# Sliding-window attention with 32-query groups: own 128-key spans and shared global keys instead of 256 score columns a tile

## The reference

```python
# q, k, v: [2, 8, 768, 64]; n_global = 8, n_local = 96
scores = q @ k.T / 8
rel = pos[:, None] - pos[None, :]
is_global = pos[None, :] < n_global
is_local = (rel >= 0) & (rel < n_local)
dist = where(is_global & ~is_local, n_local, abs(rel))
scores = where(is_global | is_local, scores - slope[head] * dist, -1e9)
a = softmax(scores); x = a @ v                  # then [2, 768, 512]
u = x + mix over the sequence (rank 32: U, V)
y = u + relu(u @ w_ch1) @ w_ch2
k2 = relu(shift_k(y) @ w_k); out = sigmoid(shift_r(y) @ w_r) * (k2 * k2 @ w_v)
```

## Time and profile before

| | us |
|---|---|
| Median of three runs | 542.37 (542.26 to 542.88) |
| The profiled execution, its device time | 543.66 |
| Its span in the profile | 541.9 |
| PE busy | 525.9 (97%) |
| DVE, ACT, POOL busy | 196.2, 133.5, 264.8 |
| First score matmul; end of the attention's last weigh | 9.16; 102.19 |

### The profile page before, as it was taken

One profiled execution on the slowest core, in us unless ns is written; L12 is line 12 of the kernel. 1 busy time (PEld: TensorE's weight loads), 2 busy tenths in 40 slices (PEclk: granted clock), 3 DMA queues, 4 the chain that ended last, 5 costly groups with the idle time before them and its releaser, 6 DMA issues.

```text
span 541.9 us, 9496 instructions
## 1 busy us (share of the span) xinstructions
PE 525.9 (97%) x3600; PEld 490.0 (90%) x3600; DVE 196.2 (36%) x529; ACT 133.5 (25%) x288; POOL 264.8 (49%) x282
## 2 busy tenths in 40 slices
PE   3989999999999999999999999999999999999997
PEld 2777787899999999999999999999998998998996
DVE  4866777422322212222122321232342342343223
ACT  2756676311111111111111101112321321321321
POOL 4489454338002700039910369930797797698000
PEclk9999999999999999999999999999999999999999
DMA  8643336002200300004420000000001001001001
GB/s 208 231 151 100 91 88 187 3 0 84 73 0 0 130 26 0 0 0 156 155 77 0 0 1 1 0 0 0 1 1 58 0 0 58 1 0 58 0 0 58
DMA packets 24602, 27.06 MB, mean 50 GB/s; under 512 B 14208, under 2 KB 14208, under 8 KB 24576
## 3 DMA queue, kind: packets, MB, share of 16 engines
q1 hardware_dynamic: 24288, 25.93, 15.0%
q10 hardware_dynamic: 288, 0.79, 0.5%
HBM read 23.57 MB, written 3.15 MB: 49 GB/s over the span
## 4 chain that ended last, share of the span: by engine, by line
PE 92%; POOL 4%; issue 1%; DMA 1%; DVE 0%; POOLq 0%; DVEq 0%
PE bank L500 25%; PE bank L512 25%; PE bank L556 12%; PE bank L565 12%; PE bank L580 6%; PE bank L365 4%; PE bank L398 3%; PE bank L373 3%; PE bank L406 1%; POOL w1l L1012 1%; POOL w2l L1012 1%; DMA v_in<-in_v 1%; PE bank L415 1%; PE bank L412 1%; POOL q_in L967 0%
## 5 line engine op out<-in xcount | busy, mean ns | idle before, releaser
L883 DVE SCALAR_TENSOR_TENSOR HL<-bank,HH 128x384 fp32r<-128x384 f32 x64 | 35.7, 558 | 175.0 <-ACT HH L687 175.0
L687 ACT ACTIVATE HH<-bank 128x384 fp32r<-128x384 f32 x64 | 31.5, 493 | 234.4 <-PE bank L500 234.4
L500 PE MATMUL bank<-UL,w1h 128*128 (+1 forms) x256 | 85.9, 336 | 0.8 <-issue 0.8
L500 PE MATMUL bank<-UH,w1h 128*128 (+1 forms) x256 | 86.4, 337 | 0.0
L512 PE MATMUL bank<-HH,w2h 128*128 128x384 f32 x256 | 86.2, 337 | 0.0
L512 PE MATMUL bank<-HL,w2h 128*128 128x384 f32 x256 | 86.2, 337 | 0.0
L500 PE MATMUL bank<-UH,w1l 128*128 (+1 forms) x256 | 86.1, 336 | 0.0
L512 PE MATMUL bank<-HH,w2l 128*128 128x384 f32 x256 | 85.9, 335 | 0.0
L1010 POOL TENSOR_SCALAR w1h<-raw 128x2048 fp32r<-128x2048 f32 x5 | 9.6, 1922 | 126.2 <-PE bank L512 126.2
L610 ACT ACTIVATE probs<-probs,neg_max 128x256 f32<-128x256 f32 (+1 forms) x96 | 41.0, 480 | 32.8 <-DVE neg_max L768 32.8
L500 PEld LDWEIGHTS bank<-UH,w1h 128*128 128x128 f32 x256 | 48.1, 188 | 1.1 <-issue 1.0
(11 more groups left out here) (110 smaller groups left out, 987.9 us busy)
## 6 DMA issues: line engine op xcount, KB each, us to landing
raw<-in_moe_w_ch SPq DMA_DIRECT2D x8, 1024.0 KB, 6.2
v_in<-in_v SPq DMA_DIRECT2D x8, 384.0 KB, 4.0
out<-result SPq DMA_DIRECT2D x12, 256.0 KB, 2.1
q_in<-in_q SPq DMA_DIRECT2D x7, 384.0 KB, 4.7
k_in<-in_k SPq DMA_DIRECT2D x7, 384.0 KB, 5.4
raw<-in_moe_w_v SPq DMA_DIRECT2D x2, 1024.0 KB, 5.3
raw<-in_moe_w_k SPq DMA_DIRECT2D x2, 1024.0 KB, 5.0
raw<-in_moe_w_r SPq DMA_DIRECT2D x1, 1024.0 KB, 5.6
```

Source lines behind the costliest of these rows:

```text
L500: mm = pe.matmul(bank[4 + f % 2][:, 0:BLK], w[:, kt, f * P:(f + 1) * P], x[:, kt, ds(blk * BLK, BLK)], start=kt == 0 and n == 0, stop=kt = ...
L687: act.activation(HH[:, f % 2, :], bank[4 + f % 2][:, 0:BLK], ACT.Relu).then_inc(hid_high, 1)
L883: dve.scalar_tensor_tensor(out=HL[:, f % 2, :], in0=bank[4 + f % 2][:, 0:BLK], scalar=0.0, in1=HH[:, f % 2, :].bitcast(F32), op0=ALU.max, ...
```

## The change

Each group of 32 queries gets a span of 128 keys of its own (its 32 and the 96 before), read straight from k, which now lies in memory with 96 zero columns ahead; the 32 global keys are scored apart. So a tile has 160 score columns: 32 of globals and 128 of the span. A score matmul has 32 queries as weights and 64 rows: 8 array tiles (2 heads by 4 groups). v comes from memory in four copies, each shifted by 32 rows (`v_in[:, slot, j, t, h, :]`), and the globals' v as `v_glob`; POOL copies neither k nor v any more. The probabilities of the four (tile, head) blocks' global columns are gathered by ACT into one 128x128 block, so that a unit has 5 transpositions. Row sums come from the exponential's accumulator. Scores, transposed blocks and products have two PSUM banks each, without alternation; `scores(n)` waits for the maxima of n-1, and `turn(n)` for both evacuations of n-1.

```diff
-                        mm = pe.matmul(bank[UNIT_BANKS[n % 3][h]][:, at:at + w].rearrange("p (a n) -> p a n", n=P),
-                                       q_in[r, p % 2, t * P:(t + 1) * P], window(p % 2, r, t), start=True, stop=True)
+                if n >= 1:
+                    pe.wait_ge(max_done, 2 * n)
+                for i, t in unit_tiles(n):
+                    for at, w in ((BAND, GLOB), (None, P)):
+                        for j in range(GROUPS):
+                            for h in range(2):
+                                r = slice(h * D, (h + 1) * D)
+                                frm = t * P + j * GROUP if at is None else at
+                                to = i * WIN + (GLOB if at is None else 0)
+                                mm = pe.matmul(bank[SCORE_BANKS[h]][group(j), to:to + w],
+                                               q_in[r, p % 2, t * P + j * GROUP:t * P + (j + 1) * GROUP],
+                                               k_in[r, p % 2, frm:frm + w], start=True, stop=True)
...
+            def turn(n):
+                if n >= 1:
                     for i in range(2):
+                        pe.wait_ge(ptevac[i], n)
                 for h in range(2):
                     pe.wait_ge(exp_done, 2 * n + h + 1)
+                    for i in range(2):
+                        mm = pe.transpose(bank[TURN_BANKS[h]][:, i * P:(i + 1) * P],
+                                          probs[:, n % 2, i, h, GLOB:WIN], ident[:, :])
+                mm.then_inc(pt_done, 1)
+                pe.wait_ge(glob_kept, n + 1)
+                pe.transpose(bank[TURN_BANKS[0]][:, 2 * P:3 * P],
+                             probs_glob[:, n % 2, :], ident[:, :]).then_inc(pt_done, 1)
...
+            def weigh_globals(n):
...
+                for j in range(GROUPS):
+                    for i in range(2):
+                        r = slice(i * 2 * GLOB, (i + 1) * 2 * GLOB)
+                        pe.matmul(WEIGHTED[group(j), i, :], probs_t[r, n % 2, 2, group(j)],
+                                  v_glob[r, p % 2, :, :].rearrange("p h d -> p (h d)"), start=True, stop=False)
+            def weigh(n):
...
+                    for i, t in unit_tiles(n):
+                        for j in range(GROUPS):
+                            mm = pe.matmul(WEIGHTED[group(j), i, h * D:(h + 1) * D],
+                                           probs_t[:, n % 2, turned_at(i, h), group(j)],
+                                           v_in[:, p % 2, j, t, h, :], start=False, stop=h == 1)
...
             def sums_of_x(x):
                 for t in range(ST):
-                    side = slice(t % 2 * 2 * RANK, (t % 2 + 1) * 2 * RANK)
-                    mm = pe.matmul(bank[M_BANK][side, 0:P], U2[:, t, :, :].rearrange("p a r -> p (a r)"), x(t),
+                    for side in (t % 2, t % 2 + 2):
+                        mm = pe.matmul(bank[M_BANK][side * RANK:(side + 1) * RANK, 0:P], U[:, t, :], x(t),
...
             def banded_attention():
-                for n in range(NU + 3):
+                for n in range(1, NU + 3):
                     if 2 <= n < NU + 2:
                         turn(n - 2)
+                    if piece(n) and piece(n)[1] > 0:
+                        mixing(*piece(n))
                     if n < NU:
                         scores(n)
-                    if piece(n):
-                        mixing(*piece(n))
                     if n >= 3:
+                        weigh_globals(n - 3)
+                        if piece(n) and piece(n)[1] == 0:
+                            mixing(*piece(n))
                         weigh(n - 3)
+            scores(0)
```

`scores(0)` now stands ahead of the branch. ACT:

```diff
-                for i, (_, at, w) in enumerate(unit_tiles(n % UNITS)):
-                    pr = probs[:, n % 3, h, at:at + w]
-                    e = act.activation(pr, pr, ACT.Exp, bias=neg_max[:, n % 3, h, i:i + 1], scale=-1.0)
+                for i in range(2):
+                    pr = probs[:, n % 2, i, h, :]
+                    e = act.activation(pr, pr, ACT.Exp, bias=neg_max[:, n % 2, i, h:h + 1], scale=-1.0,
+                                       accum_out=sums[:, n % 4, i, h:h + 1])
                 e.then_inc(exp_done, 1)
+            def keep_globals(n):
+                act.wait_ge(exp_done, 2 * n + 2)
+                act.activation(probs_glob[:, n % 2, :].rearrange("p (a g) -> p a g", g=GLOB),
+                               probs[:, n % 2, :, :, 0:GLOB].rearrange("p i h g -> p (i h) g"),
+                               ACT.Copy).then_inc(glob_kept, 1)
```

```diff
             def load_v(p):
-                sp.dma_start(v_in[:, p % 2, :, :, 0:D], vp[p]).then_inc(v_landed[p % 2], 16)
+                sp.dma_start(v_in[:, p % 2, :, :, :, :], vp[p]).then_inc(v_landed[p % 2], 16)
+                sp.dma_start(v_glob[:, p % 2, :, :], vg[p]).then_inc(v_landed[p % 2], 16)
...
             for p in range(2, PAIRS):
                 sp.wait_ge(qk_done, UNITS * (p - 1))
                 sp.wait_ge(qk_in[p % 2], 32 * (p // 2))
                 load_qk(p)
                 sp.wait_ge(pv_done, UNITS * (p - 1))
-                sp.wait_ge(v_landed[p % 2], 16 * (p // 2))
+                sp.wait_ge(v_landed[p % 2], 32 * (p // 2))
                 load_v(p)
+                if p < 4:
+                    load_chunk(p - 2)
...
+            act.dma_start(q_in[:, 0, 0:FIRST], qt[0][:, 0:FIRST]).then_inc(first_in, 16)
+            act.dma_start(k_in[:, 0, 0:BAND + FIRST], kt_[0][:, 0:BAND + FIRST]).then_inc(first_in, 16)
...
                 for p in range(PAIRS):
                     if p + 2 < PAIRS:
-                        prepare_qk(p + 2)
+                        prepare_pair(p + 2)
                     if p >= 1:
                         split_u(p - 1, 0)
                         split_u(p - 1, 1)
-                    if p + 2 < PAIRS:
-                        prepare_v(p + 2)
-                    if p < 2:
-                        split_chunk(p)
+                    if 1 <= p < 3:
+                        split_chunk(p - 1)
```

More of the change, by code:

```diff
@@ L19, with block_kernel @@
 GLOB = 32
-BAND = P - GLOB
+GROUP = 32
+BAND = P - GROUP
 MASK = 1.0e9
-def block_kernel(nc, qt, kt_, vp, counts, mix_u, mix_v, w_ch1, w_ch2, mus, w_k, w_v, w_r, out):
+def block_kernel(nc, qt, kt_, vp, vg, counts, mix_u, mix_v, w_ch1, w_ch2, mus, w_k, w_v, w_r, out):
     PAIRS, _, S = qt.shape
-    D = vp.shape[4]
+    D = vp.shape[5]
     B, H = out.shape[0], out.shape[2] // D
@@ L143, in block_kernel @@
         v_rows = region("v_rows", [P, S])
-        u_raw = region("u_raw", [P, ST, RANK])
-        region = Region(h_at)
-        dist = region("dist", [P, BCOLS])
-        grid = region("grid", [P, 2 * P])
-        far = region("far", [P, 2 * P])
+        region = Region(y_at)
+        reach = region("reach", [P, 2, WIN])
+        far = region("far", [P, 2, WIN])
+        grid = region("grid", [P, P])
+        place = region("place", [P, P])
+        behind = region("behind", [P, P])
         key = region("key", [P, GLOB])
         glob_far = region("glob_far", [P, GLOB])
+        region = Region(h_at)
+        dist = region("dist", [P, 2, WIN])
+        v_glob = region("v_glob", [P, 2, 2, D])
+        probs_glob = region("probs_glob", [P, 2, P])
         assert region.at <= b_at
@@ L177, in block_kernel @@
         assert end <= nc.sbuf_usable_end, (end, nc.sbuf_usable_end)
[L179 to L183 removed]
+        psum = ctx.enter_context(nc.psum_tensor("psum", [P, 8, 512], F32))
+        bank = [psum[:, i, :] for i in range(8)]
+        WEIGHTED = psum[:, 0:2, 0:2 * D]
+        TURN_BANKS, SCORE_BANKS = (2, 3), (4, 5)
+        M_BANK = 7
         GATE_BANKS = [4, 5, 3]
@@ L333, in _ @@
             sp.dma_start(mu[:, :, :], mus).then_inc(mu_in, 16)
-            for c in range(2):
-                sp.dma_start(raw[c][:, :].rearrange("p (t n) -> p t n", t=4), chunks[c][0]).then_inc(raw_in[c], 16)
             for p in range(2, PAIRS):
@@ L727, in _ @@
                                 -SCALE / slopes[2 * j + h]).then_inc(scale_set, 1)
+            for j in range(GROUPS):
+                dve.memset(group_base[group(j), :], float(j * GROUP)).then_inc(reach_step, 1)
+            reaches()
             dve.wait_ge(counts_in, 16)
@@ L1105 @@
         "q": inputs["q"].transpose(0, 1, 3, 2).reshape(pairs, 2 * d, s),
-        "k": inputs["k"].transpose(0, 1, 3, 2).reshape(pairs, 2 * d, s),
-        "v": inputs["v"].reshape(pairs, 2, tiles, P, d).transpose(0, 3, 2, 1, 4),
+        "k": np.pad(inputs["k"].transpose(0, 1, 3, 2).reshape(pairs, 2 * d, s), ((0, 0), (0, 0), (BAND, 0))),
+        "v": np.zeros((pairs, P, P // GROUP, tiles, 2, d), inputs["v"].dtype),
+        "v_glob": np.zeros((pairs, 2, 2, GLOB, 2, d), inputs["v"].dtype),
         "counts": np.concatenate([np.asarray(inputs[n]).reshape(1) for n in ("n_local", "n_global")]),
     }
+    v = inputs["v"].reshape(pairs, 2, s, d)
+    ahead = np.pad(v, ((0, 0), (0, 0), (BAND, 0), (0, 0)))
+    for j in range(P // GROUP):
```

(5 more changed lines are left out.)

283 lines of the change are left out of this document (124 added, 159 removed).

## The result

The changed kernel takes 568.95 us (567.62 to 570.11, 4 runs) against 542.62 for the kernel before in the same session: ratio 1.0485, 95% interval 1.046 to 1.0509. The forecast was 529.2, and the range of 523 to 552 misses it. The profiled execution took 570.11, its span is 568.6. Times here are medians of executions, without those over 1.5% above the kernel's fastest (two of w6's, four of w8's, two of x15's; the 548.0 in later expectations is w8's median with them).

The account below looks back on a forecast made before the run. PE was taken to bound every stage, its streams in attention to shrink: -10.3 + 0.9 - 1.9 - 0.9 - 1.0 = -13.2 us, from 543.66 profiled to 530.5, or 529.2 as median; range 523 to 552.

Parts of the forecast that it names:

- PE, part by part: Attention, steps 6 to 23: a pair takes PE 9.55 us instead of 11.27, six pairs -10.3 us.
- my 0.007: Globals' scores on PE: estimated 0.007 us for a matmul start, weights included; 32 starts, 0.22 us.
- Starts are the limit: Rival, chance 0.20: attention's many small matmuls start only every 0.029 us, so the kernel is slower, 566 us.
- Do the others keep up: Attention: whether DVE, ACT, POOL and loads keep to 3.18 us a step; stalls 3.5 instead of 2.57, +0.9 us.
- The clock falls: Rival, chance 0.03: small idle times put PE's array at 1.2 GHz for part of attention; 550 us and more.
- the forecast's savings after step 3: Attention: -10.3 us for PE in six pairs, -0.9 for steps 4 and 5, -1.0 for steps 24 to 26.
- Start: Attention to the end of step 3: first scores some 1.5 us earlier than 9.16; -1.9 us in all.
- Even if the smaller loads land no earlier: Start: less scaling and no copying of k ahead of the first scores gain some 1.5 us without earlier loads.
- ScalarE binds: Rival, chance 0.12: accumulator reads of 0.255 us make ACT's attention step 3.45 with waits; 5 us slower than forecast, 534.
- my ends of 0.083 and 0.255: ACT's accumulator read after each exponential: 0.083 us taken, like DVE's; 0.255, a whole small instruction, in the rival.
- Loads bind: Rival, chance 0.09: at 307 GB/s a pair's q and k come 1.2 us late in attention; 538 us.
- The new waits: Attention: scores behind the previous maxima, turn behind evacuations and keep_globals; all three costed at nothing.

Follow-up runs that it names:

- w6: e3 with 16 identity matmuls on PE ahead of the first scores; 550.77 us.
- w8: w6 with v of pair 0 issued behind the mixing's factors and q and k of pair 1; 546.74 us.
- x15: x14 with v of pairs 2 to 7 loaded as in the changed kernel, but only one of its four copies (results wrong); 546.25 us.
- e3: Changed kernel with the globals' scores and products in one matmul for 128 queries instead of four for 32; 555.06 us.
- e4: Kernel before with scores and products cut into groups of 32 queries, same streamed columns and loads; 547.97 us.
- w5: Changed kernel with 16 identity matmuls on PE ahead of the first scores; 576.99 us.
- e1: Changed kernel with each pair's v loaded in four transfers at once instead of one, same bytes; 567.28 us.
- x13: Changed kernel with v's four copies loaded one by one, spread over three steps, same bytes; 564.97 us.
- e2: Changed kernel with only one of v's four copies loaded from pair 2 on (results wrong); 560.36 us.
- x14: w8 with v's loads spread over three steps and two early PE gaps filled with 5 and 2 identity matmuls; 550.40 us.
- x17: x14 with v's loads spread over two steps instead of three; 551.06 us.
- x11: w8 with PE's gaps ahead of the scores of units 1 and 2 filled with 10 and 5 identity matmuls; 551.28 us.

## Why the prediction was wrong

- **PE, part by part (-10.3): right in what it priced.** Scores 0.74 (forecast 0.90), weigh_globals 0.41 (0.26), step with mixing 3.08 (3.15). For a whole pair no stretch without stops exists; e3's, 10.71, less the 0.42 by which its scores are longer, three times, is 9.45 (estimate; forecast 9.55). Starts lie 0.74 / 64 = 0.0116 apart on average, streams included, far under the 0.029 of the rival; less the span's 0.43, 32 starts have 0.31, under 0.010 each, beside my 0.007. The Trainium skill (TensorE: Matmul & The Clock Gate, Part 1) has about 25 ns for the distance of two starts; 64 in 0.74 us on eight array parts, and e4's 64 in 1.06, differ. *Starts are the limit* named the sign and nearly the time (566), by a mechanism that the runs refute.
- **"Do the others keep up": the step that failed.** I asked it of DVE, ACT, POOL and the loads, and not of what feeds PE itself. The sum has no term for instructions, though I had counted 112 matmuls for a step where there were 40, and the page of before had the queue (16 packets). The term measures 22.1 us of stops. A count of instructions a step against the 3.7 us of a page would have given it, though that figure comes from the changed kernel's trace: 257 / 256 x 3.7 = 3.7 us a step instead of 3.2, 18 x 0.5 = 9, and up to 6 x 3.3 = 20 more where a pair's loads delay every third page from 3.7 to 7 us; the 22.1 lie between.
- **The clock falls (0.03): underweighted, and not independent.** It falls with the stops (31 us at 1.2 GHz with 22.1 of stops, 51 with 30.0 in w5, none in e4 with 4.1). Attention grew by 25.6; the stops are 22.1, and the forecast's savings after step 3, -10.3 - 0.9 - 1.0, are to be had only at the full clock, so 25.6 - 22.1 + 12.2 = 15.7 are left for the low clock and the start. That is worked out by difference; at w8's price, 8 us for 24, the 31 us at 1.2 GHz are some 10 of it (estimate).
- **Start (-1.9): wrong.** 9.84 instead of 7.6. "Even if the smaller loads land no earlier" is what failed: they land later, behind v(0). w8, with v(0) moved, starts at 7.94; e1 and x13, with the same v(0) in four transfers of 3 KB rows, at 6.42, for the first keys land at 5.7 instead of 9.1.
- **ScalarE binds: no.** The read takes 0.187, between my ends of 0.083 and 0.255; ACT's step would be 3.0, and it has no wait of PE to its name. Exponential 0.417 (0.42), maxima 0.321 (0.32) as forecast.
- **Loads bind: no** wait for q_in beside the start, but they do their harm in a way that I hadn't listed, by holding up pages. (The sum had the bytes slightly wrong: 1536, 64 and 816 KB are 2.47 MB, not 2.52, and v's part is 1.64, not 1.68; a tenth of a us.)
- **The new waits at nothing:** nearly right, 1.2 us in all for the maxima, once, ahead of the second unit's scores.
- **Still open:** how much of 569 is v's burst (e1, e2 and x13 give 2, 9 and 4 us), why the clock falls in some executions of w8 and not in others, and stays down for 23.5 us without a wait, and whether the form with 32-query groups can win once pages, v and the jump are all on time. None of the runs got it under the kernel before; w8's executions at the full clock (542.9 to 544.6) equal it, with e3's longer scores, which cost 24 x 0.42 = 10 us against the changed kernel's (estimate).

## What to carry to other kernels

Before cutting matmuls into smaller ones, count the instructions of the busiest engine by stage, weight loads too, and divide by 256: with some 4 us of work in a page or less, or 7 where large loads run beside it, expect stops (the packets' distances here; at 4.6 us a page e4 had four, at 4.9 e3 none and w8 four), and nothing in the profile of before shows it but the packets of the instruction queue. A cut that streams fewer columns with twice the instructions isn't a gain in itself; here the shortest way back was fewer and larger matmuls. Stops in the midst of one kind of matmul, released by nothing, at a fixed distance in instructions (the sequencer's counted too), are its sign.

## What was unexpected of the hardware

- PE's instructions come in pages of 256, and in small matmuls too slowly: packets start 3.4 to 4.1 us apart at best, take 0.9 to 1.4, and PE goes on 1.2 to 1.5 after one has landed. Stops reach 3.5 us (4.4 in w5).
- Beside a pair's loads (2.5 MB) a packet comes 6.4 to 7.6 us after the last one.
- Adding 64 instructions at the start of a program moved all later stops and made it 8 us slower (w5).
- The array stayed at 1.2 GHz for 23.5 us of work without a wait in w8's profile, and at 2.4 GHz in other executions of the same program (granted clock 0.977 and 1.000, 551.6 and 543 to 545 us), and in x11, whose two gaps of 1.3 and 0.6 us were filled.
- The first matmul behind the jump after the attention stopped PE for 3.1 to 3.6 us in three runs (x14, x15, x17) and for under 0.5 in nine; what decides it is open.
